# The other-limits branch placed first, the usual one second, and the flag read ahead of the bias

## What is computed

```python
# attention: batch 2, heads 8, seq 768, head_dim 64; n_global = 8, n_local = 96
scores = q @ k.T / sqrt(D)
keep = (pos_k < n_global) | ((rel >= 0) & (rel < n_local))
scores = where(keep, scores - slope[h] * dist, -1e9)
attn = softmax(scores) @ v                      # -> x [1536, 512]
# top-1 of 8 experts: cosine logits / tau, gate = softmax probability of the chosen one
out[mask] = gate_w[mask] * (relu(x[mask] @ w1[e]) @ w2[e])      # 512 -> 1024 -> 512
# dense mixture of 4 experts
out += p[:, e] * (relu(x @ w1[e]) @ w2[e])
```

## Time and profile before

| | us |
|---|---|
| median of 3 runs | 923.72 (922.93 to 924.23) |
| span of the profiled execution | 920.3 |
| TensorE busy | 864.0 (94%) |
| VectorE busy | 317.8 (35%) |
| ScalarE busy | 219.6 (24%) |
| GpSimd busy | 288.0 (31%) |
| first L703 (bias and maximum) | 11.76 |
| last attention matmul on TensorE ends | 133.49 |
| first scatter | 143.69 |
| first expert matmul L1133 | 167.34 |

### The profile page before, as it was taken

How to read it: one execution, slowest core, us unless ns; L and a number is a source line. 1 busy time by engine, 2 the same in 40 slices (tenths; PEclk the granted TensorE clock), 3 DMA queues, 4 the chain that set the end, 5 groups by cost and what they waited for, 6 DMA issues and landing times.

```text
span 920.3 us, 12898 instructions
## 1 busy us (share of the span) xinstructions
PE 864.0 (94%) x4433; PEld 697.1 (76%) x4434; DVE 317.8 (35%) x775; ACT 219.6 (24%) x476; POOL 288.0 (31%) x162
## 2 busy tenths in 40 slices
PE   7898862899999999899999999999999999999998
PEld 5566542688887788788888888888888888888886
DVE  7888772344434434122221212121212121212212
ACT  3777580013333333212101111111111111111110
POOL 5363415027778877550000370000740000500000
PEclk9999995999999999999999999999999999999999
DMA  6799643126667766540000140000220000001001
GB/s 243 226 310 308 201 137 138 35 70 210 207 197 228 227 193 194 176 146 1 1 0 0 42 142 0 0 0 0 92 91 1 0 0 0 1 0 46 19 26 46
DMA packets 33075, 90.96 MB, mean 99 GB/s; under 512 B 4232, under 2 KB 4616, under 8 KB 33040
## 3 DMA queue, kind: packets, MB, share of 16 engines
q1 hardware_dynamic: 23056, 54.86, 17.9%
q10 hardware_dynamic: 8064, 29.36, 10.1%
q0 software_dynamic: 1920, 6.29, 2.1%
HBM read 72.67 MB, written 17.83 MB: 98 GB/s over the span
## 4 chain that ended last, share of the span: by engine, by line
PE 81%; DMA 6%; DVE 5%; issue 4%; POOL 1%; ACT 1%; SPq 1%; DVEq 0%; ACTq 0%
PE ps L1207 28%; PE ps L1194 28%; PE ps L1151 10%; PE ps L1133 7%; DMA xg<-x_sorted 3%; PE ps L1018 2%; DMA win<-qkv 1%; PE ps L1006 1%; POOL x_sorted L472 1%; PE ps L1032 1%; PE ps L1141 1%; PE ps L1123 1%; ACT arena L527 1%; PE ps L977 1%; DVE den L722 1%
## 5 line engine op out<-in xcount | busy, mean ns | idle before, releaser
L1207 PE MATMUL ps<-ring,h 128*128 128x512 f32 x1152 | 275.9, 390 | 0.0
L1194 PE MATMUL ps<-ring 128*128 (+1 forms) x864 | 256.4, 389 | 0.0
L277 POOL TENSOR_TENSOR ring<-raw,ring 128x1024 fp32r<-128x1024 f32 x96 | 227.7, 2396 | 83.7 <-ACT ring L272 80.8
L1207 PEld LDWEIGHTS ps<-ring,h 128*128 128x128 f32 x1152 | 215.7, 188 | 44.6
L945 DVE SCALAR_TENSOR_TENSOR h<-ps,h 128x512 fp32r<-128x512 f32 x96 | 66.3, 691 | 366.3 <-ACT h L596 366.3
L1194 PEld LDWEIGHTS ps<-ring 128*128 128x128 f32 x864 | 162.0, 188 | 33.8 <-DVE x2b L938 0.2
L596 ACT ACTIVATE h<-ps 128x512 fp32r<-128x512 f32 x96 | 57.6, 600 | 427.3 <-PE ps L1194 427.3
L272 POOL CAST ring<-raw 128x1024 fp32r<-128x1024 f32 x36 | 37.5, 1043 | 381.5 <-PE ps L1194 321.2
L1194 PE MATMUL ps<-x2b,ring 128*128 (+1 forms) x288 | 112.1, 389 | 0.0
L272 ACT CAST ring<-raw 128x1024 fp32r<-128x1024 f32 x60 | 62.2, 1052 | 176.1 <-PE ps L1151 116.2
L1133 PE MATMUL ps<-ring,xT 128*128 x384 | 91.5, 394 | 0.8 <-DVE xT L898 0.6
(11 more groups left out here) (115 smaller groups left out, 528.4 us busy)
## 6 DMA issues: line engine op xcount, KB each, us to landing
raw<-wts ACTq DMA_DIRECT2D x56, 512.0 KB, 4.2
raw<-wts SPq DMA_DIRECT2D x40, 512.0 KB, 3.8
win<-qkv SPq DMA_DIRECT2D x32, 320.0 KB, 4.3
x_sorted<-ring SPq DMA_DIRECT2D x20, 256.0 KB, 5.0
xg<-x_sorted SPq DMA_DIRECT2D x17, 256.0 KB, 3.4
y_sorted<-yrow SPq DMA_DIRECT2D x16, 256.0 KB, 3.9
win<-qkv SPq DMA_DIRECT2D x8, 384.0 KB, 6.1
result<-xrow SPq DMA_DIRECT2D x12, 256.0 KB, 2.1
```

Source lines behind the costliest of these rows:

```text
L277: nc.gpsimd.tensor_tensor(w_part(u, 1)[:, q * CW:q * CW + CW], raw[:, q, :], w_part(u, 0)[:, q * CW:q * CW + CW].bitcast(F32), ALU.subtrac ...
L1194: ins = nc.tensor.matmul(ps[:, 4 + f % 2, :], w_part(u1, wp)[:, k * F + f * P:k * F + f * P + P], x2T(xp, k)[:, bass.ds(g * 512, 512)], st ...
L1207: ins = nc.tensor.matmul(ps[:, t, :], h2[:, f % 2, hp_, t * P:t * P + P], w_part(u1 + 1, wp)[:, f * DM:f * DM + DM], start=(f == 0 and n = ...
```

## The change

In all four programs with a branch, the condition becomes `fast < 1`, the general path is the first body and the usual path is the `Else`. What an engine does in either path stays, with these exceptions:

- VectorE: squaring the embeddings and building the bias are made functions and called behind the branch (the general path calls only the first), so the flag is read before them.
- TensorE: `keep_busy(32)` becomes `keep_busy(8)`; the `Else` begins with a `keep_busy(24)` of its own; the wait for the identity moves behind the branch. The `keep_busy(24)` after the first scores stays. `keep_embeddings` accordingly waits for three rounds of `keep_busy` and not two.
- ScalarE: the general path no longer waits for `bias_built`.
- SyncE: the two bodies change places, nothing else.

```diff
             fast = flag_of(sp)
-            with sp.If(fast > 0):
+            with sp.If(fast < 1):
...
             fast = flag_of(act)
-            with act.If(fast > 0):
...
-            with act.Else():
-                act.wait_ge(bias_built, 1)
+            with act.If(fast < 1):
                 act.dma_start(g_rel0, consts[:, 3 * P + 2 * C3:3 * P + 2 * C3 + S]).then_inc(rel0_ready, 16)
...
+            with act.Else():
+                def exp_probs(hp, i):
...
             nc.vector.tensor_copy(flag_i[:, :], flag[:, 2:3]).then_inc(flag_ready, 1)
 
-            dve.wait_ge(emb_ready, 16)
-            nc.vector.tensor_tensor_reduce(out=embq_t, in0=emb_t, in1=emb_t, scale=1.0, scalar=0.0,
-                                           op0=ALU.mult, op1=ALU.add, accum_out=norm_e[:, 0:1]).then_inc(emb_sq, 1)
...
+            def square_embeddings():
...
+            def build_bias():
...
-            def keep_embeddings(idle_times=2):
+            def keep_embeddings(idle_times=3):
...
             before_paths = done[0]
             fast = flag_of(dve)
-            with dve.If(fast > 0):
...
+            with dve.If(fast < 1):
+                square_embeddings()
                 scale_embeddings()
                 keep_embeddings(1)
                 expert_weights()
...
+            with dve.Else():
+                done[0] = before_paths
+                square_embeddings()
+                build_bias()
...
             pe.wait_ge(idle_ready, 1)
-            keep_busy(32)
+            keep_busy(8)
...
-            pe.wait_ge(ident_ready, 16)
             fast = flag_of(pe)
-            with pe.If(fast > 0):
...
-            with pe.Else():
+            with pe.If(fast < 1):
+                pe.wait_ge(ident_ready, 16)
                 turn_embeddings()
...
+            with pe.Else():
+                keep_busy(24)
+                pe.wait_ge(ident_ready, 16)
```

More of the change, by code:

```diff
@@ L398, in _ @@
             order = [(pair, w) for pair in range(1, HP * B) for w in range(NW)]
-            with sp.If(fast > 0):
+            with sp.If(fast < 1):
+                for m, (pair, w) in enumerate(order):
+                    if w or pair > 1:
+                        sp.wait_ge(x_written, pair * TQ)
+                        load_window(pair, w)
+                    beside_attention(m)
+            with sp.Else():
                 for m, (pair, w) in enumerate(order):
@@ L408, in _ @@
                         load_window(pair, 0)
[L409 to L415, removed]
                     beside_attention(m)
@@ L521, in _ @@
             fast = flag_of(act)
-            with act.If(fast > 0):
+            with act.If(fast < 1):
+                act.dma_start(g_rel0, consts[:, 3 * P + 2 * C3:3 * P + 2 * C3 + S]).then_inc(rel0_ready, 16)
+                with act.Fori(0, HP) as hp:
+                    for m in range(2 * DUO):
+                        act.wait_ge(g_biased, hp * (2 * DUO) + (m + 1))
+                        nc.scalar.activation(g_t, g_t, ACT.Exp, bias=g_sc[:, 4:5],
+                                             accum_out=g_sc[:, 5:6]).then_inc(g_probs, 1)
+                for t in range(NT):
+                    squares(HP - 1, t)
+                norms()
+            with act.Else():
                 def exp_probs(hp, i):
@@ L545, in _ @@
                          closing={squares: 5}, after={DUO + 2: load_roots})
-                norms()
-            with act.Else():
-                act.wait_ge(bias_built, 1)
[L549 to L556, removed]
                 norms()
@@ L625, in _ @@
             nc.vector.tensor_copy(flag_i[:, :], flag[:, 2:3]).then_inc(flag_ready, 1)
-            dve.wait_ge(emb_ready, 16)
-            nc.vector.tensor_tensor_reduce(out=embq_t, in0=emb_t, in1=emb_t, scale=1.0, scalar=0.0,
-                                           op0=ALU.mult, op1=ALU.add, accum_out=norm_e[:, 0:1]).then_inc(emb_sq, 1)
[L632 to L636, removed]
-            nc.vector.tensor_tensor(bias[:, 0, :], slope_t, mask_t, ALU.add)
-            nc.vector.scalar_tensor_tensor(bias[:, 1, :], slope_t, 0.5, mask_t, ALU.mult, ALU.add).then_inc(bias_built, 1)
-            dve.wait_ge(bias_built, 1)
+            def square_embeddings():
+                dve.wait_ge(emb_ready, 16)
+                nc.vector.tensor_tensor_reduce(out=embq_t, in0=emb_t, in1=emb_t, scale=1.0, scalar=0.0,
+                                               op0=ALU.mult, op1=ALU.add, accum_out=norm_e[:, 0:1]).then_inc(emb_sq, 1)
+            def build_bias():
+                dve.wait_ge(const_ready, 16)
+                step(nc.vector.tensor_scalar(mask_t, rel_t, nl, None, ALU.is_lt))
+                step(nc.vector.scalar_tensor_tensor(mask_t, key_t, ng, mask_t, ALU.is_lt, ALU.max))
+                nc.vector.tensor_scalar(slope_t, rel_t, nl, -0.5 / SCALE, ALU.min, ALU.mult)
+                step(nc.vector.tensor_scalar(mask_t, mask_t, -1.0, 64e9 / SCALE, ALU.add, ALU.mult))
+                nc.vector.tensor_tensor(bias[:, 0, :], slope_t, mask_t, ALU.add)
+                nc.vector.scalar_tensor_tensor(bias[:, 1, :], slope_t, 0.5, mask_t, ALU.mult, ALU.add).then_inc(bias_built, 1)
+                dve.wait_ge(bias_built, 1)
             def scale_embeddings():
@@ L749, in _ @@
-            with dve.Else():
-                done[0] = before_paths
+            with dve.If(fast < 1):
+                square_embeddings()
                 scale_embeddings()
```

184 lines of the change are left out of this document (92 added, 92 removed).

## The result

The changed kernel is slower. Over 20 runs of each on one chip its median is 925.28 us (920.79 to 930.34) against 923.10 us (917.59 to 926.91), a ratio of **1.0032 with a 95% interval of 1.0017 to 1.0047**, so 3.0 us more (1.6 to 4.3). The ratio is that of the means, 925.65 and 922.67; the medians differ by 2.2. What was forecast is +0.5 us, and what was measured is +3.0; the case held likeliest, no change that can be told (0.59), did not come. A second comparison on the chip of the first experiments gave 1.0039 (1.0017 to 1.0062).

The account below looks back on a forecast made before the run. TensorE was taken to bound the kernel (busy 94%), its later loops moving as a block. Profiled span 920.3 + 2.8 (S) - 2.35 (G) = 920.8; the median lies 3.4 above the span, hence 924.2 us, range 921.4 to 925.9.

Parts of the forecast that it names:

- the case held likeliest: Whole kernel: time between 921.9 and 925.6 us, not to be told from no change; chance 0.59.
- G: End of attention: how much earlier the routing chain begins after attention; 2.35 us, bounds 0 and 2.42.
- L838's wait for ScalarE: End of attention: with VectorE's idle time gone, L838 waits for ScalarE's L519 and can start at about 135.86.
- The far branch at the start: Kernel start: the branch, now taken, stalls VectorE 3.1 us and TensorE 3.7 us, both issuing at about 4.2.
- S: Whole attention: how much later it runs after the late start; 2.8 us, bounds 1.6 and 4.6.
- the slower rival: Start: second scores after about 18.5, L645 misses its slot, S 4.6 to 5.5, time 926.0 to 926.9; chance 0.10.
- The bias: VectorE's start: six operations take 4.66 us behind the branch and the square, done at 12.7 instead of 10.69.
- These four quarters come at fixed times: Early attention: GpSimd's weight quarters (12.24 to 26.4) don't move with attention, so a late attention meets fewer of them.
- TensorE's start: Behind TensorE's branch: 24 low-pace warm-up matmuls take 4.9 to 5.1 us; first scores at 12.95, second at 16.3.
- TensorE wouldn't stall: Start: TensorE's branch target is held already, so S is 0.1 and the time 921.5; chance 0.12.
- nothing would happen: Both ends: falling through costs as much, G = 0, no stall at the start, 923 to 924.5; chance 0.04.
- Slower: Whole kernel: time above the border of 925.6, from the slower rival and the likeliest rival's upper end; chance 0.17.

Follow-up runs that it names:

- the end alone: Kernel before, with VectorE's routing chain written into both bodies ahead of the branch out; ratios to before 0.9965 and, run again, 0.9979.
- the kernel held without its loads: Changed kernel, with SyncE issuing all loads except limits and embeddings only after VectorE's embedding square; one time, 928.67 us, against 925.35 for the median of before.

## Why the prediction was wrong, point by point

**The end: right.** G = 2.35 was put together from the idle time, the root and the step that waits for it; the trace shows 2.3, two comparisons of the end alone average 2.6 (intervals: gains of 1.2 to 5.3, and from a loss of 0.2 to a gain of 4.1). That L838's wait for ScalarE would be next is what happened.

**The far branch at the start: right in kind, wrong in size.** This is the step that failed: the stall of a taken far branch, 3.1 us on VectorE and 3.7 on TensorE in the sum, measured 5.2 and 5.8, and with it S was put at 2.8 us and measured about 5.3. The 3.1 and 3.7 us were taken from branches at the end of attention, where nothing else was in flight, and the loads at 4 to 8 us were allowed for only as an upper bound ("if the fetch takes 1.3 us more in the loaded queues") and as a condition of the slower rival. They cost 2.1 us more on both engines. The row that warned stood in the prediction: a DMA share of 1.06 in just that stretch. A price read in a stretch with free queues was carried to one with full queues. No run changes this price alone, so that it accounts for all of the missing 2.5 us of S is argued; the parts that the traces show follow.

**The bias: not foreseen.** The prediction let the six operations take the 4.66 us of before and end at 12.7. With VectorE resuming at 7.3 it would by the same rows have been done before the first L277 (13.36 before); 2.2 us later the last two ran into GpSimd, and the bias ended at 17.6. The rule was at hand, it had been applied to L645 and L722 and not to the bias; in the kernel before L637 and L638 never met an L277. "These four quarters come at fixed times" fell with it: they gave as well as they took, with L277 at 18.60 and 25.69 instead of 16.97 and 24.05.

**TensorE's start: right but for the branch.** The 24 matmuls at the low pace were put at 4.9 to 5.1 and took 5.30; the scores came at 15.28 and 19.02 instead of 12.95 and 16.3, 2.1 of it from the branch, the rest from the 24 and from first scores of 1.08 us and not 0.70. The working behind the pace is weaker than it looks: 22 x 0.213 + 10 x 0.11 is 5.79 and not 5.98, and the low pace was tied to a granted clock of 0.50, while the same rows grant 1.00 at 4 to 8 us, where part of the 32 ran at the low pace. The 0.22 us are measured; why the granted clock doesn't show them stays open. ScalarE's root and table load slid too (10.22 and 11.46), and cost nothing, as foreseen: its branch over the shorter general body, recorded at 11.0, was followed by the table load 0.46 us later, and its first exponential came at 18.47.

**What reaches the end: too much given back.** The start of each unit's first operation, us:

| unit | before | predicted | measured | measured shift |
|---|---|---|---|---|
| 1 | 11.76 | 13.65 (scores done) | 17.66 | 5.9 |
| 2 | 12.45 | 17.05 | 19.77 | 7.3 |
| 3 | 16.30 | 20.6 | 21.61 | 5.3 |
| 4 | 19.26 | 23.05 | 24.57 | 5.3 |
| 5 | 23.05 | 27.3 | 28.36 | 5.3 |
| 6 | 26.34 | 29.0 | 29.64 | 3.3 |
| 7 | 27.63 | 31.05 | 31.97 | 4.3 |
| 11 | 36.48 | 39.25 | 40.66 | 4.2 |

The giving back is there, but smaller than foreseen: 5.3 us at the third to fifth unit become 4.3 at the seventh and 4.2 at the eleventh. The 3.3 at the sixth is only a moment. That unit followed the fifth by 1.28 us, its scores waiting; the seventh had to wait for its own scores (31.15 to 31.85) and came 2.33 us later, where in the kernel before it came 1.29 later. The prediction carried the sixth unit's lead on in steps of 2.05, 10.25 us to the eleventh. The kernel before takes 10.14 for them and the changed one 11.02, and this difference comes from the seventh unit's step. (`expert_weights`, L667 to L671, which the prediction doesn't count, lengthens the step behind the seventh in both kernels, to 3.17 and 2.92.) So of the 1.4 us missing at the eleventh unit, 0.6 is there at the sixth, and the rest comes in with the two steps behind it, for which 2.05 was too little. What lies between the 4.2 of this trace and the 5.3 of the comparisons can't be placed; the second trace of the changed kernel has 5.1 at the eleventh unit.

From the eleventh unit on nothing more is given back, on average over the traces: the five kernels with an undisturbed start have it at 34.45 to 36.87 (mean 36.0) and the 48th unit at 125.67 to 127.85 (127.2); the six with a late start at 40.54 to 43.16 (41.7) and 129.67 to 135.09 (132.7). That is 5.7 us at one, 5.5 at the other, and it agrees with the 5.3 of the comparisons. The trace of the changed kernel is at the low end of its group, which its start doesn't explain; the kernel held without its loads is left out of the count.

**The rivals.** The slower one, with 0.10, was right in its condition and its size. A fetch over 1.5 us dearer held (2.1), as did the second scores after 18.5 (19.02). Its S of 4.6 to 5.5 is what was measured, and its 926.0 to 926.9 take in 923.72 x 1.0032 = 926.7. But its path to that size is not what happened: L645 was to miss its slot and wait to 23.0, and it slipped in (20.82, 0.47 us), because L277 had moved too. So the agreement in size is in part luck. The slot was missed in the kernel with VectorE's program of before. That TensorE wouldn't stall, and that nothing would happen, is refuted by the branch record and by the vanished idle time. The Trainium skill, "Runtime: NRT & Kernel Launch", section "Instruction fetch mechanics", has a taken branch with a target not held fetch first; the trace agrees for VectorE's and TensorE's far branches, with a fetch packet behind each and 5.2 and 5.8 us of stall. The same section's room for 2,048 instructions on TensorE didn't save the stall at the start, with a target some 1,600 on.

**The chances.** "Slower" stood at 0.17. The fetch's price was the one term whose bounds came from a different state of the queues, and it moved S across the border; the sum's own working says that a dearer fetch of 1.5 us is enough. With the loaded stretch taken at its word, that case should have had a larger share; how much larger is a judgement that no run settles. The signs named for being wrong lay on the fast side (TensorE resuming before 6, second scores before 16, L645 before 16.97) or at the end, and none came up. What did show was the branch of 5.8 us against the 3.5 to 5 that were said, and the bias operations starting at 10.12 and not near 8; the eleventh unit, 40.66, lay within its 38.1 to 41.1.

## What to carry to other kernels

Read the price of an operation in a stretch whose queues are as full as where it will stand; here the fetch for a far branch came 2.1 us later with loads in flight. Where two engines feed each other at the start, ask for each delay what it is hidden by: here neither's removal gave the start back, and of the starts tried only those without a far branch on either engine kept their time. And if a jump at the end of a stage is what costs, put the next chain of work ahead of the jump, in both bodies, instead of moving the jump to a place where everything waits.

## What the runs showed that was not expected

- A taken branch to far code costs 2.9 to 3.1 us on VectorE and 3.6 to 3.7 us on TensorE with free DMA queues, and 5.1 to 5.4 and 5.3 to 5.8 us while loads fill them. A branch that isn't taken costs 0.05 to 0.1 us. Code fallen into at the end of a body cost nothing that shows.
- VectorE's operations on 128x768 with two large inputs are slowed by GpSimd's casts and subtractions, not only the small tensor_scalar ones: L637 0.96 to 1.67, L638 0.95 to 3.10 us. With TensorE's program of before, two with one input were too: L635 0.62 to 1.49, L636 0.55 to 2.69. And GpSimd's L277 itself went from 2.35 to 2.93 beside them.
- The same program's traces differ by 5.4 us at the 48th unit (129.67 and 135.09) with the first and the third to seventh unit alike within 0.2 us, so a question of 3 us needs the comparisons, or stages averaged over several traces.
